# A fused attention, expert routing and two-layer kernel: the second products one block later, the high halves first, and the splitting work at other places

## The chip, the cores and the metric

The kernel is one program on one core of a Trainium2 chip. Five engines work side by side: PE (TensorE, matmuls), DVE (VectorE), ACT (ScalarE), POOL (GpSimd) and SP (SyncE, which here only issues transfers). They wait for each other through semaphores. The metric is the device time of one execution in microseconds (us), the median over the runs; a lower number is better.

## What is computed

```python
# attention with decay, over B=4 batches, H=8 heads, S=768 steps, D=48
for t in range(S):
    cur = einsum('bhd,bhe->bhde', u[None] * kt, vt)
    y[:, :, t] = einsum('bhd,bhde->bhe', rt, state + cur)
    state = w[None, :, :, None] * state + einsum('bhd,bhe->bhde', kt, vt)
x = y.transpose(0, 2, 1, 3).reshape(3072, 384)
# expert layer: 8 experts of exactly 384 tokens, given out by descending logit
logits = x @ w_gate
for idx in argsort(-logits.flatten()):
    tok, e = idx // 8, idx % 8
    if assigned[tok] >= 0 or counts[e] >= 384: continue
    assigned[tok] = e; counts[e] += 1
for e in range(8):
    out[assigned == e] = relu(x[assigned == e] @ w1[e]) @ w2[e]      # 384 -> 1024 -> 384
# common layer
h = relu(out @ w_in)                                                 # 384 -> 2048
out = (h * h) @ w_out                                                # 2048 -> 384
```

## The kernel before

**Attention** goes over 24 units (6 chunks of 128 steps, 4 batches each). For each unit the tensor engine makes the scores, the part from the state and the part inside the chunk; DVE adds them to a row tile `yrow` (`rows`). One unit later `turn` transposes this tile into PSUM bank 6 (`tr_ps`), ACT copies it to `yT` (`turned_y`), `gate` multiplies it with `w_gate` into the end of the same bank (`lg_ps`), and ACT copies the eight logits (`gated`). Since one bank serves all units, `turn` waits until the logits of the unit before have been copied out (`logit_ready`).

**Routing.** Experts are not filled token by token. For the expert that fills up next a threshold on the keys (the logit's bits) is searched in six steps: DVE compares all keys with a ramp of thresholds (`keys`, then `compare`, written to `hot`), the tensor engine counts (`count`), DVE tests the counts (`fullness`), and the tensor engine adds up the result (`add_full`), which the next compare needs. Then `ranks`, `slots`, `slot_hot` and `slot_ids` turn the winners into 384 row numbers (`perm`), and POOL gathers the rows with an indirect DMA (`gather`). The first search stands alone, between attention and the experts. The other six are done during the work of the expert before: five of them in a loop, the last expert needs no search at all.

**Expert stages.** There are eight, which I number 0 to 7. In each, blocks g = 0 to 7 are the expert's own layer and g = 8 to 23 the common layer. `hidden(g)` makes 128 rows of the hidden layer, `contract(g)` multiplies them by the second matrix and adds to three accumulator banks. Every float32 value is split into a high part (what the fast format holds) and a low part (the rest), and each product is made of three matmuls: high times high, high times low, low times high (`three`). One `hidden` or `contract` is thus nine matmuls of 384 columns. ACT makes the high part `h_hi` (`high`), DVE the low part `h_lo` (`low`); for g of 8 and above DVE makes the square `sq` and POOL the low part. Block 24 of a stage is block 0 of the next one.

**What sets the order.** It is written out by hand in one loop over g for each engine, and each engine does its instructions strictly in that order. In the search stages the tensor engine does `count` number g-2 behind block g, for g = 2 to 7, and `add_full` number g-3 inside `hidden(g)`. DVE's loop begins at g = 1 with `low`, `need`, `keys` and the first `compare`.

**Splitting the weights.** Each expert's weights are six tiles of 128 x 1024 in three buffers: SP loads them, ACT makes `w_hi` (`split_high`), DVE `w_lo` (`split_low`). Tiles 0 to 2 are the first matrix (W1_TILES = 3). The common second matrix is split once, in stage 0: `out_low` makes one of twelve halves of 128 x 512 (`m_lo`), and the table `OUT_LOW_AT` says behind which g each stands.

`fill` is a run of matmuls whose result nobody reads; it stands where the tensor engine would idle.

## Time and profile before

| | |
|---|---|
| median of 3 runs | 811.03 us (810.62 to 811.88) |
| the profiled execution: its own time, and its span | 812.36 us, 810.6 us |
| busy in the span: PE, DVE, ACT, POOL | 777.7, 500.7, 321.5, 292.9 us |
| instructions | 19168 |
| mean granted clock of the tensor engine | 0.978 of full |
| tensor engine's part of the chain that ended last | 79% (DVE 10%, "issue" 4%, POOL 3%) |

The span is the time from the first to the last instruction; what the profiled execution's time has beyond it (1.76 us) lies around it. The chain that ended last is the work, followed back from the last instruction, in which each piece released the next. The granted clock is what the chip's throttle gave the tensor engine, 1.00 being the upper of its two levels (2.4 GHz) and 0.50 the lower (1.2 GHz).

### The profile page before, as it was taken

The numbers are of one execution on the slowest core, as the hardware profiler recorded it, in microseconds if no ns is written. First come the engines' busy times: TensorE is split into PE (matmuls) and PEld (weight loads), VectorE is DVE, ScalarE is ACT, GpSimd is POOL, SyncE is SP. The second block draws the span as 40 slices with busy tenths as digits, with TensorE's granted clock in tenths as the row PEclk, the third lists the DMA queues.
The fourth block names the chain that finished last, engine by engine and source line by source line (L and its number), as shares of the span: only waits on it lengthen the run. The fifth ranks groups of instructions, "written<-read, shape, count | busy, mean of one in ns | idle before, by whom it ended". The sixth has DMA issues, their size and how long they took to land.

```text
span 810.6 us, 19168 instructions
## 1 busy us (share of the span) xinstructions
PE 777.7 (96%) x6971; PEld 743.8 (92%) x6971; DVE 500.7 (62%) x1195; ACT 321.5 (40%) x718; POOL 292.9 (36%) x295
## 2 busy tenths in 40 slices
PE   8999994799999999999999999999999999999996
PEld 6999993589899999999999999999999999999995
DVE  7988886788846783678367837783777336721210
ACT  4556654313532353235323532363236324531332
POOL 7766640102631163116311631263126312621333
PEclk9999996699999999999999999999999999999998
DMA  8878744502300140013001300130013002300000
GB/s 227 263 233 239 236 126 177 183 3 79 108 1 30 40 145 0 29 49 136 0 29 51 133 0 29 55 129 0 29 56 128 0 30 79 108 1 30 0 1 30
DMA packets 22196, 65.27 MB, mean 81 GB/s; under 512 B 3664, under 2 KB 6736, under 8 KB 22160
## 3 DMA queue, kind: packets, MB, share of 16 engines
q1 hardware_dynamic: 19088, 55.34, 21.4%
q0 software_dynamic: 3072, 9.44, 3.3%
q8 instruction: 24, 0.39, 0.2%
q14 instruction: 12, 0.10, 0.0%
HBM read 55.33 MB, written 9.44 MB: 80 GB/s over the span
## 4 chain that ended last, share of the span: by engine, by line
PE 79%; DVE 10%; issue 4%; POOL 3%; ACT 1%; DMA 1%; POOLq 0%; SPq 0%; DVEq 0%; ACTq 0%
PE bank L1362 14%; PE bank L1366 14%; PE bank L1363 14%; PE bank L1420 7%; PE bank L1421 7%; PE bank L1422 7%; PE bank L1166 3%; PE bank L1204 3%; PE bank L1179 3%; DVE hot L863 2%; DVE hot L977 1%; PE bank L1233 1%; PE bank L1220 1%; PE bank L1241 1%; POOL xg L476 1%
## 5 line engine op out<-in xcount | busy, mean ns | idle before, releaser
L503 POOL TENSOR_TENSOR h_lo<-sq,h_hi 128x384 fp32r<-128x384 f32 x128 | 155.4, 1217 | 377.3 <-DVE sq L1076 377.2
L1076 DVE SCALAR_TENSOR_TENSOR sq<-bank,relu 128x384 f32<-128x384 f32 x128 | 71.0, 555 | 152.1 <-ACT relu L627 150.1
L627 ACT ACTIVATE relu<-bank 128x384 f32<-128x384 f32 x128 | 62.9, 492 | 196.1 <-PE bank L1366 182.5
L1420 PE MATMUL bank<-m_hi,h_hi 128*128 128x384 f32 x384 | 132.7, 346 | 2.2 <-POOL h_lo L503 2.0
L1362 PE MATMUL bank<-x_hi,m_hi 128*128 128x384 f32 x384 | 129.8, 338 | 0.6
L1421 PE MATMUL bank<-m_lo,h_hi 128*128 128x384 f32 x384 | 130.2, 339 | 0.0
L1366 PE MATMUL bank<-x_hi,m_lo 128*128 128x384 f32 x384 | 130.0, 339 | 0.0
L1422 PE MATMUL bank<-m_hi,h_lo 128*128 128x384 f32 x384 | 129.8, 338 | 0.0
L1363 PE MATMUL bank<-x_lo,m_hi 128*128 128x384 f32 x384 | 128.9, 336 | 0.0
L621 ACT ACTIVATE h_hi<-bank 128x384 fp32r<-128x384 f32 x64 | 31.5, 492 | 175.3 <-PE bank L1366 175.3
L1068 DVE SCALAR_TENSOR_TENSOR h_lo<-bank,h_hi 128x384 fp32r<-128x384 f32 x64 | 35.4, 554 | 73.2 <-ACT h_hi L621 73.2
L1420 PEld LDWEIGHTS bank<-m_hi,h_hi 128*128 128x128 f32 x384 | 72.3, 188 | 4.5 <-POOL h_lo L503 4.5
L1362 PEld LDWEIGHTS bank<-x_hi,m_hi 128*128 128x128 f32 x384 | 72.3, 188 | 2.0 <-DVE x_lo L1096 0.9
L1421 PEld LDWEIGHTS bank<-m_lo,h_hi 128*128 128x128 f32 x384 | 72.5, 189 | 0.0
L1422 PEld LDWEIGHTS bank<-m_hi,h_lo 128*128 128x128 f32 x384 | 72.4, 189 | 0.0
L1366 PEld LDWEIGHTS bank<-x_hi,m_lo 128*128 128x128 f32 x384 | 72.3, 188 | 0.0
L1363 PEld LDWEIGHTS bank<-x_lo,m_hi 128*128 128x128 f32 x384 | 72.3, 188 | 0.0
L629 ACT ACTIVATE h_hi<-relu 128x384 fp32r<-128x384 f32 x128 | 67.2, 525 | 4.0
L1362 PE MATMUL bank<-x_hi,w_hi 128*128 128x384 f32 x192 | 67.3, 351 | 0.5 <-DVE x_lo L1030 0.5
L1366 PE MATMUL bank<-x_hi,w_lo 128*128 128x384 f32 x192 | 67.2, 350 | 0.0
L1362 PE MATMUL bank<-h_hi,w_hi 128*128 128x384 f32 x192 | 64.5, 336 | 1.4 <-DVE h_lo L1068 1.4
L294 DVE TENSOR_TENSOR w_lo<-w_raw,w_hi 128x1024 fp32r<-128x1024 f32 x48 | 63.9, 1334 | 2.1 <-ACT w_hi L597 2.1
(191 smaller groups left out, 1445.3 us busy)
## 6 DMA issues: line engine op xcount, KB each, us to landing
w_raw<-we_in SPq DMA_DIRECT2D x48, 512.0 KB, 5.5
nn<-nn_in SPq DMA_DIRECT2D x24, 384.0 KB, 4.0
tt<-tt_in SPq DMA_DIRECT2D x44, 192.0 KB, 4.3
m_raw<-m_in SPq DMA_DIRECT2D x12, 512.0 KB, 6.1
x_rows<-yrow SPq DMA_DIRECT2D x24, 192.0 KB, 2.2
tt<-tt_in SPq DMA_DIRECT2D x4, 256.0 KB, 5.9
xg<-x_rows,perm_next POOLq DMA_INDIRECT x24, 5.1
out<-xg,perm_now POOLq DMA_INDIRECT x24, 2.6
```

Of the source, the lines that this page charges most:

```text
L294: eng.tensor_tensor(w_lo[:, cols], w_raw[j % W_SLOTS][:, :], w_hi[:, cols].bitcast(f32), ALU.subtract).then_inc(w_lo_ready, 1)
L503: pool.tensor_tensor(h_lo[g % 3][:, :], sq[g % 2][:, :], h_hi[g % 3][:, :].bitcast(f32), ALU.subtract).then_inc(lo2_ready, 1)
L627: act.activation(relu[:, :], h_ps[g % 3][:, 0:CAP], ACT.Relu).then_inc(relu_ready, 1)
L629: act.activation(h_hi[g % 3][:, :], relu[:, :], ACT.Square).then_inc(h_hi_ready, 1)
L1068: dve.scalar_tensor_tensor(out=h_lo[g % 3][:, :], in0=h_ps[g % 3][:, 0:CAP], scalar=0.0, in1=h_hi[g % 3][:, :].bitcast(f32), op0=ALU.max, ...
L1076: dve.scalar_tensor_tensor(out=sq[g % 2][:, :], in0=h_ps[g % 3][:, 0:CAP], scalar=0.0, in1=relu[:, :], op0=ALU.max, op1=ALU.mult).then_inc ...
L1362: pe.matmul(out, hi_w, hi_x, start=first, stop=False)
L1363: pe.matmul(out, hi_w, lo_x, start=False, stop=False)
L1366: return pe.matmul(out, lo_w, hi_x, start=False, stop=last)
L1420: pe.matmul(acc_ps[t][:, 0:DM], h_hi[r][:, s], m2_hi[:, c:c + DM], start=first, stop=False)
L1421: pe.matmul(acc_ps[t][:, 0:DM], h_hi[r][:, s], m2_lo[:, c:c + DM], start=False, stop=False)
L1422: last = pe.matmul(acc_ps[t][:, 0:DM], h_lo[r][:, s], m2_hi[:, c:c + DM], start=False, stop=end)
```

## The change

Six edits.

1. `turn` and `gate` of attention's last unit write to bank 7 (`u_ps`), so that `turn` no longer waits for the logits of the unit before, but for the last state.
2. The keys of the first 20 units are made ahead of the last `rows`, not behind it.
3. The gathered rows of stage 0 are transposed into the accumulator banks instead of the hidden banks, and `fill` uses bank 2.
4. In the expert's own layer `contract` stands two blocks behind `hidden` instead of one, and the last three stand together behind block 7.
5. `hidden` of g = 0 and g = 8 waits for the high half of its input only; the low half is waited for in front of the last of the three products.
6. In stage 0 the three splits of the second matrix stand behind `high(0, 0)` and `low(0, 0)`, and at g = 2 and 4; the twelve `out_low` are placed anew.

```diff
-OUT_LOW_AT = [2, 3, 4, 5, 8, 10, 13, 15, 16, 17, 18, 19]
+OUT_LOW_AT = [8, 8, 8, 10, 10, 10, 17, 17, 18, 18, 19, 19]
...
+        def turned_in(n):
+            return u_ps if isinstance(n, int) and n == NU - 1 else tr_ps
+        def gated_in(n):
+            return turned_in(n)[:, 504:512]
...
-            return (h_ps[d] if is_first(q) else rt_ps if d == 1 else xt_ps)[:, 0:CAP]
+            return (acc_ps[d] if is_first(q) else rt_ps if d == 1 else xt_ps)[:, 0:CAP]
...
             high(0, 0)
-            for j in range(W1_TILES + 1, WE_TILES):
+            for j in range(W1_TILES, WE_TILES):
                 split_high(0, j)
...
                     if last and b == B - 1:
                         pick(slice(0, EARLY), begin=False)
                         need()
+                        keys(slice(0, EARLY))
                     rows(i, b)
...
-                        if is_first(i) and g == 3:
-                            split_low(dve, 0, W1_TILES + 2)
-                        if is_first(i) and g in OUT_LOW_AT:
-                            out_low(dve, OUT_LOW_AT.index(g)).then_inc(out_lo_ready, 1)
+                        if is_first(i) and g in (2, 4):
+                            split_low(dve, 0, W1_TILES + g // 2)
+                        if is_first(i):
+                            for n in range(2 * OUT_TILES):
+                                if OUT_LOW_AT[n] == g:
+                                    out_low(dve, n).then_inc(out_lo_ready, 1)
...
             low(0, 0)
-            split_low(dve, 0, W1_TILES + 1)
+            split_low(dve, 0, W1_TILES)
...
+                elif turned_in(n) is tr_ps:
+                    pe.wait_ge(logit_ready, n)
                 else:
-                    pe.wait_ge(logit_ready, n)
+                    pe.wait_ge(state_ready, NU)
...
                 pe.matmul(out, hi_w, hi_x, start=first, stop=False)
+                if low_ready:
+                    pe.matmul(out, lo_w, hi_x, start=False, stop=False)
+                    pe.wait_ge(*low_ready)
+                    if between:
+                        between()
+                    return pe.matmul(out, hi_w, lo_x, start=False, stop=last)
...
                         if g == 0:
                             pe.wait_ge(w_lo_ready, WE_TILES * i + d + 1)
-                            pe.wait_ge(x_lo_ready, DC * i + d + 1)
+                            pe.wait_ge(x_hi_ready, DC * i + d + 1)
+                            low_ready = x_lo_ready, DC * i + d + 1
...
                         if g == G1:
-                            pe.wait_ge(x2_lo_ready, DC * i + d + 1)
+                            pe.wait_ge(x2_hi_ready, DC * i + d + 1)
+                            low_ready = x2_lo_ready, DC * i + d + 1
...
-                    if g < G1:
+                    if 1 < g < G1:
+                        contract(i, g - 2)
+                    if g == G1 - 1:
                         contract(i, g - 1)
-                    if g == G1 - 1:
                         contract(i, g)
```

**The tensor engine at the head of an expert stage.** Its rows from the top of the loop to the first half of the first count; a row is `line operation output<-inputs columns`, a `hidden` reads `x_hi,w_hi`, a `contract` reads `h_hi,w_hi`, and "..." stands for the other eight matmuls of each. Before:

```order
L1462 UNCONDITIONAL_BRANCH
L1362 MATMUL bank<-x_hi,w_hi 128x384
...
L1362 MATMUL bank<-h_hi,w_hi 128x384
...
L1362 MATMUL bank<-x_hi,w_hi 128x384
...
L1362 MATMUL bank<-h_hi,w_hi 128x384
...
L1300 MATMUL bank<-need,ones 128x8
L1303 REGISTER_ALU
L1304 MATMUL bank<-openc,hot 128x16 x6
```

And of the changed kernel:

```order
L1483 UNCONDITIONAL_BRANCH
L1373 MATMUL bank<-x_hi,w_hi 128x384
...
L1373 MATMUL bank<-x_hi,w_hi 128x384
...
L1373 MATMUL bank<-h_hi,w_hi 128x384
...
L1311 MATMUL bank<-need,ones 128x8
L1314 REGISTER_ALU
L1315 MATMUL bank<-openc,hot 128x16 x6
```

Between the loop's head and the first count stood four groups of nine matmuls; now three. The missing one, a `contract`, stands behind the last block of the expert's layer.

**DVE in stage 0, blocks 8 to 11.** `sq` is the square of a block, `m_lo` an `out_low`, `cand<-r` the last step of `filled` (g = 9), on which `ranks` waits. Before:

```order
L1076 SCALAR_TENSOR_TENSOR sq<-bank,relu 128x384
L288 TENSOR_TENSOR m_lo<-m_raw,m_hi 128x512
...
L938 TENSOR_REDUCE cand<-r 128x24
L1076 SCALAR_TENSOR_TENSOR sq<-bank,relu 128x384
L288 TENSOR_TENSOR m_lo<-m_raw,m_hi 128x512
L1076 SCALAR_TENSOR_TENSOR sq<-bank,relu 128x384
L943 SCALAR_TENSOR_TENSOR pre<-ones,bank 128x48
```

And of the changed kernel:

```order
L1082 SCALAR_TENSOR_TENSOR sq<-bank,relu 128x384
L296 TENSOR_TENSOR m_lo<-m_raw,m_hi 128x512 x3
...
L946 TENSOR_REDUCE cand<-r 128x24
L1082 SCALAR_TENSOR_TENSOR sq<-bank,relu 128x384
L296 TENSOR_TENSOR m_lo<-m_raw,m_hi 128x512 x3
L1082 SCALAR_TENSOR_TENSOR sq<-bank,relu 128x384
L951 SCALAR_TENSOR_TENSOR pre<-ones,bank 128x48
```

Four more halves stand in front of the routing's `slots` (line 943 before) and `slot_hot`; in exchange there is none any more at blocks 2 to 5, 13, 15 and 16.

## Rows read from the trace of the kernel before

**Rows 1.** Work by stretch of time: busy time (x count) per engine, granted clock.
```profile
core 0: us, PE busy (x) PEld busy (x) DVE busy (x) ACT busy (x) POOL busy (x), PEclk, DMA share, GB/s
158.00:168.10 10.10, 8.50 (x57) 7.94 (x58) 7.07 (x15) 4.33 (x6) 0.00 (x0) 1.00 0.37 141
...
219.30:222.80 3.50, 3.50 (x12) 3.50 (x13) 3.42 (x3) 0.53 (x1) 1.72 (x2) 0.51 0.07 28
231.00:311.70 80.70, 80.59 (x531) 77.86 (x530) 51.02 (x130) 30.33 (x56) 26.93 (x23) 1.00 0.15 54
```
**Rows 2.** Weight loads of the tensor engine in time, stage 1: start, length, ..., [idle before].
```profile
246.76 0.19 PEld L1362 LDWEIGHTS bank<-x_hi,w_hi 128*128 128x128 f32 x1
...
251.45 0.19 PEld L1362 LDWEIGHTS bank<-h_hi,w_hi 128*128 128x128 f32 x1
...
253.18 0.10 PEld L1300 LDWEIGHTS bank<-need,ones 128*128 128x128 bf16 x1 [0.16 <-DVE key_lo L835]
...
253.51 0.19 PEld L1362 LDWEIGHTS bank<-x_hi,w_hi 128*128 128x128 f32 x1
```
**Rows 3.** ACT and DVE in order of time in the same stretch of stage 1.
```profile
248.70 0.49 ACT L621 ACTIVATE h_hi<-bank 128x384 fp32r<-128x384 f32 x1 [1.08 <-PE bank L1366]
...
251.17 1.83 DVE L867 TENSOR_TENSOR hot<-key_hi,ramps 128x768 bf16<-128x768 int32 x2
```
**Rows 4.** Stage 0 in order of time, from the last weight tile to the first count.
```profile
162.66 0.19 PEld L1362 LDWEIGHTS bank<-h_hi,w_hi 128*128 128x128 f32 x1 [1.74 <-issue]
...
162.88 1.06 ACT L597 ACTIVATE w_hi<-w_raw 128x1024 fp32r<-128x1024 f32 x1 [0.85 <-DMA w_raw<-we_in]
...
166.09 1.83 DVE L867 TENSOR_TENSOR hot<-key_hi,ramps 128x768 bf16<-128x768 int32 x2
...
167.97 0.21 PEld L1304 LDWEIGHTS bank<-openc,hot 128*128 128x128 bf16 x6 [0.27 <-DVE hot L867]
...
168.11 0.19 PEld L1362 LDWEIGHTS bank<-x_hi,w_hi 128*128 128x128 f32 x1
```
**Rows 5.** The tensor engine's waits in stage 0 behind the first count, timeline.
```profile
177.69 0.11 PEld L1312 LDWEIGHTS bank<-full,ones_times 128*128 128x128 bf16 x2 [1.06 <-DVE folded L889]
...
181.66 0.10 PEld L1312 LDWEIGHTS bank<-full,ones_times 128*128 128x128 bf16 x1 [0.50 <-DVE folded L889]
```
**Rows 6.** Timeline row of stage 0; then waits of the whole span: us, times, longest.
```profile
219.15 0.19 PEld L1420 LDWEIGHTS bank<-m_hi,h_hi 128*128 128x128 f32 x1 [2.27 <-POOL h_lo L503]
...
PEld bank L1420 <- POOL h_lo L503: 4.5, 7, 2.3
```
**Rows 7.** POOL in order of time, gather and next low part, stages 0 and 1.
```profile
212.09 1.62 POOL L476 DMA_INDIRECT xg<-x_rows,perm_next  x1 [0.99 <-DVE open_t L1008]
...
218.10 2.92 POOL L503 TENSOR_TENSOR h_lo<-sq,h_hi 128x384 fp32r<-128x384 f32 x3
...
295.77 1.59 POOL L476 DMA_INDIRECT xg<-x_rows,perm_next  x1 [1.04 <-DVE open_t L1008]
...
300.19 2.14 POOL L503 TENSOR_TENSOR h_lo<-sq,h_hi 128x384 fp32r<-128x384 f32 x2
```
**Rows 8.** DVE and weight loads in stage 0, blocks 8 to 14; last, the halves grouped.
```profile
192.38 0.68 DVE L288 TENSOR_TENSOR m_lo<-m_raw,m_hi 128x512 fp32r<-128x512 f32 x1
...
193.37 0.56 DVE L1076 SCALAR_TENSOR_TENSOR sq<-bank,relu 128x384 f32<-128x384 f32 x1 [0.32 <-ACT relu L627]
...
196.74 0.35 DVE L938 TENSOR_REDUCE cand<-r 128x24 bf16<-128x192 f32 x1
...
197.35 0.10 PEld L1321 LDWEIGHTS bank<-cand,before 128*128 128x128 bf16 x1 [0.16 <-issue]
...
206.92 0.67 PEld L1328 LDWEIGHTS bank<-ids,hot 128*128 128x128 bf16 x24 [0.16 <-DVE hot L977]
...
L288 DVE TENSOR_TENSOR m_lo<-m_raw,m_hi 128x512 fp32r<-128x512 f32 x12 | 10.2, 851 | 0.0
```
**Rows 9.** The tensor engine's last turn in attention, timeline.
```profile
124.63 0.52 PE L1233 MATMUL bank<-ident,yrow 128*128 128x128 f32 x3 [0.43 <-ACT logits L546]
```
**Rows 10.** Weight load at block 8 of stage 6, where nothing is counted.
```profile
674.23 0.19 PEld L1362 LDWEIGHTS bank<-x_hi,m_hi 128*128 128x128 f32 x1 [0.45 <-DVE x_lo L1096]
```

More of the change, by code:

```diff
@@ L223, in build @@
         sc_ps, y_ps, tr_ps, u_ps = bank[0:2], [banks[:, 2 + 2 * j:4 + 2 * j, :] for j in range(2)], bank[6], bank[7]
-        lg_ps, own_ps = tr_ps[:, 504:512], tr_ps[:, 496:504]
+        own_ps = tr_ps[:, 496:504]
+        def turned_in(n):
+            return u_ps if isinstance(n, int) and n == NU - 1 else tr_ps
+        def gated_in(n):
+            return turned_in(n)[:, 504:512]
         h_ps, acc_ps, rt_ps, xt_ps = bank[0:3], bank[3:6], bank[6], bank[7]
@@ L540, in turned_y @@
                     act.wait_ge(logit_sum, n)
-                act.activation(yT[:, :], tr_ps[:, 0:DM], ACT.Copy).then_inc(yT_ready, 1)
+                act.activation(yT[:, :], turned_in(n)[:, 0:DM], ACT.Copy).then_inc(yT_ready, 1)
             def gated(n):
                 act.wait_ge(logit_sum, n + 1)
-                act.activation(logits[:, bass.ds(n, 1), :].rearrange("p o e -> p (o e)"), lg_ps,
+                act.activation(logits[:, bass.ds(n, 1), :].rearrange("p o e -> p (o e)"), gated_in(n),
                                ACT.Copy).then_inc(logit_ready, 1)
@@ L614, in _ @@
                 x_high(0, d)
-            split_high(0, W1_TILES)
             def high(i, g):
@@ L1030, in x_low @@
                 dve.tensor_tensor(x_lo[:, d, :], turned(q, d), x_hi[:, d, :].bitcast(f32), ALU.subtract).then_inc(x_lo_ready, 1)
-            keys(slice(0, EARLY))
             compare(0, 0, "a")
@@ L1061, in _ @@
                 x_low(0, d)
-            split_low(dve, 0, W1_TILES)
             def low(i, g):
@@ L1228, in turn @@
                     pe.wait_ge(own_ready, 2)
+                elif turned_in(n) is tr_ps:
+                    pe.wait_ge(logit_ready, n)
                 else:
-                    pe.wait_ge(logit_ready, n)
+                    pe.wait_ge(state_ready, NU)
                 for d in range(DC):
-                    last = pe.transpose(tr_ps[:, d * P:(d + 1) * P], yrow[b][:, d * P:(d + 1) * P], ident[:, :])
+                    last = pe.transpose(turned_in(n)[:, d * P:(d + 1) * P], yrow[b][:, d * P:(d + 1) * P], ident[:, :])
                 last.then_inc(yT_sum, 1)
@@ L1240, in gate @@
                     for t in range(0, P, HALF):
-                        last = pe.matmul(lg_ps[t:t + HALF, :], yT[:, d * P + t:d * P + t + HALF], wg[:, d, :],
+                        last = pe.matmul(gated_in(n)[t:t + HALF, :], yT[:, d * P + t:d * P + t + HALF], wg[:, d, :],
                                          start=d == 0, stop=d == DC - 1)
@@ L1349, in _ @@
             slot_ids(0)
-            fill(FILLS[0], 1)
+            fill(FILLS[0], 0)
             for t in range(TT):
@@ L1357, in _, with three @@
                         last.then_inc(x_sum, 1)
-                fill(FILLS[t + 1], 1)
-            def three(out, hi_w, lo_w, hi_x, lo_x, first, last, between=None):
+                fill(FILLS[t + 1], 0)
+            def three(out, hi_w, lo_w, hi_x, lo_x, first, last, between=None, low_ready=None):
                 pe.matmul(out, hi_w, hi_x, start=first, stop=False)
+                if low_ready:
[4 more added lines that the diff above has]
+                    return pe.matmul(out, hi_w, lo_x, start=False, stop=last)
                 pe.matmul(out, hi_w, lo_x, start=False, stop=False)
@@ L1373, in hidden @@
                 for d in range(DC):
+                    low_ready = None
                     if g < G1:
@@ L1384, in hidden @@
                         if g == G1:
-                            pe.wait_ge(x2_lo_ready, DC * i + d + 1)
+                            pe.wait_ge(x2_hi_ready, DC * i + d + 1)
+                            low_ready = x2_lo_ready, DC * i + d + 1
                     last = three(h_ps[h][:, 0:CAP], w1[:, c:c + P], w2[:, c:c + P], a1[:, d, :], a2[:, d, :],
-                                 d == 0, d == DC - 1, between if d == DC - 1 else None)
+                                 d == 0, d == DC - 1, between if d == DC - 1 else None, low_ready)
                 last.then_inc(h_sum, 1)
```

## The prediction

> **What bounds the kernel now.** I read the page first: the tensor engine is busy in 777.7 of 810.6 us, and the chain of waits that ended last runs on it for 79%. So the change can only gain where the tensor engine waits, and every new wait on it costs its full length. Next I went through the tensor engine's weight loads in order of time and looked for steps longer than those inside a dense stretch. In stages 1 to 7 there is next to nothing: from 246.76 to 251.45 three groups of nine matmuls take 4.69 us, 1.56 a group or 0.174 a matmul [rows 2]. The waits are in stage 0 and at a few edges: 1.74 us ahead of its first `contract` [rows 4], 1.06 and 0.50 in its search [rows 5], 2.27 for a low part from POOL [rows 6], behind which the clock is at half for one stretch [rows 1], 0.43 at attention's last `turn` [rows 9], and 0.45 at block 8 of stage 6, and the same in stage 7, where no count fills the gap [rows 10]. That is all the change can win. The thing to look at is what waits for the tensor engine and is only just in time, for there a shifted order makes a new wait. Such a place is the first count of a stage.
>
> **The change part by part.** The sum is made against the profiled execution (812.36 us, span 810.6) and then set on the median of 811.03, which lies 1.3 lower.
>
> *Contract two blocks behind, stages 1 to 5.* The first search step of a stage hangs on `hidden(1)`: ACT makes its high part at 248.70, DVE its low part, then `need`, `keys` and the two halves of the first compare from 251.17, which end at 253.00 [rows 3]. The count is started at 253.18 [rows 2], so it came 0.2 us behind its data. Nothing in this chain moves: `hidden(1)` stands at the head of the stage as before. But there is one group of nine less between it and the count. The tensor engine is at the count at 253.18 - 1.56 = 251.62, and stands until the second half is written. From that moment to the next `hidden` stage 0 shows what it takes: end 167.92, count 167.97, next weights 168.11, 0.19 us [rows 4]. The next `hidden` then starts at 253.19 instead of 253.51, with four groups done instead of five: 1.56 - 0.32 = 1.24 us lost. The group that was left out is done behind block 7, where nothing waited for it. Behind the standing count is the whole remaining stage, each step of which (count, test, sum, compare) keeps its distance, so nothing is given back. Stages 1 to 5 have a search: 5 x 1.24 = **+6.2**. Stages 6 and 7 have none and lose nothing here.
>
> *The same in stage 0.* Here the chain to the first compare hangs on something else: `high` of block 1 stands on ACT behind the last weight tile, which comes by DMA and is split at 162.88; the compare runs from 166.09 to 167.92 [rows 4]. The changed order keeps `high(0,1)` behind that tile. So the wait of 1.74 at the first `contract` goes, but the tensor engine then stands at the count, from about 163.5 on, until the same compare. At the next `hidden` it has done one group less: **+1.6**. All this comes earlier by what attention gives, next item.
>
> *Attention's last turn.* It waited 0.43 us for the logits of the unit before [rows 9]; the state and the rows it now waits for are there. Keys ahead of the last `rows` take DVE's idle time and keep it off this chain. **-0.4**, and everything up to the first compare follows, the DMAs of gather and weights too.
>
> *Clock at the new wait.* From 163.5 to 167.5 the tensor engine has nearly nothing to do, longer than the 2.27 us behind which the clock fell [rows 6]. In that stretch 12 matmuls took 3.5 us [rows 1], at 0.174 each they take 2.1, so one such stretch costs 1.4. The 1.74 us in stage 0 did not do it: the clock is 1.00 from 158.0 to 168.1 [rows 1]. I take one stretch lost: **+1.4**; bounds 0 and 2.8.
>
> *Splits in stage 0's search.* Before there was a half at g = 2, a tile and a half at g = 3, a half at g = 4, and the waits were 1.06 (behind g = 3) and 0.50 (behind g = 4) [rows 5]. Now there is a tile at g = 2, none at 3, a tile at g = 4. A half takes 0.68 [rows 8] and a tile has twice the columns, so I take 0.6 more for it: the wait of 1.06 goes, the 0.50 becomes 1.1, and at g = 2 some 0.3 would appear but for the half clock, which gives DVE time. **-0.5**.
>
> *Twelve halves at new places.* Ahead of `ranks` and `slot_ids` in stage 0 there are now six halves instead of two, 4 x 0.68 = 2.7 us, less the 0.32 that DVE idled at 193.37: 2.4 us late. DVE had 0.26 us to spare at `ranks` (197.09 against 197.35) and the tensor engine already waited for `hot` at `slot_ids` [rows 8]. So the tensor engine waits about 2.2 us more there, in two pieces. In return no half stands beside the gather, which took 6.0 us from 212.09 to 218.10 in stage 0 and 4.4 in stage 1 [rows 7]; the wait for the low part behind it falls from 2.27 to what the other six have, (4.5 - 2.3) / 6 = 0.4 [rows 6]. Together 2.2 + 0.4 - 2.3 = **+0.3**. Bounds: -1 if DVE finds the time elsewhere, +1.3 if each half takes the mean of 0.851 [rows 8] and blocks on POOL. The pieces are shorter than the 2.27, so the half-clock stretch goes: **-1.4**.
>
> That the gather is quicker without halves beside it is what the two stages' rows show, no more. The Trainium skill (SBUF — State Buffer, Who interferes with whom) speaks against it: a DVE `tensor_tensor` with both inputs in SBUF shuts out only those GpSimd instructions that read SBUF, and it infers that writing a gather's descriptors is not among them. By the rule the gather would stay at 6.0 us, and the sum would be 1.6 higher.
>
> *High halves first.* At block 8 of stages 6 and 7 the 0.45 goes, with a little on the two blocks of input behind it 0.5 each: **-1.0**. In stages 1 to 5 the count stands there and hides it: 0. The other banks for stage 0's transposes and fills change no wait: 0. If their cover failed it would be the length of one `x_lo`, about 0.5.
>
> Sum: -0.4 + 1.6 + 1.4 - 0.5 + 0.3 - 1.4 + 6.2 - 1.0 = +6.2. On the profiled execution that is 818.6, on the median **817.2 us**, 0.8% slower.
>
> **The rivals.**
> - *Stage 0 comes out cheaper*: no clock lost at the long wait (-1.4), and half of the halves' delay hidden (-1.1). 814.7 us. The rows show 2.27 us of waiting with a fallen clock behind it and 1.74 without, and this wait is cut in two by the first half of the count. Chance 0.17.
> - *The gather is slow for another reason than DVE* (the rule above): its 6.0 us stay, +1.6, 818.8 us. For it: the first piece of the gather took 1.62 and 1.59 us in the two stages, alike with and without a half near it [rows 7]. Chance 0.13.
> - *The clock also falls at the five new waits*: each has 1.24 us of standing plus a count of tiny matmuls. Against it the 1.74 us in stage 0 that left it at 1.00. Between two and five times 1.4: 820 to 824. Chance 0.06.
> - *Faster: the count is not reached early*, because the compare comes sooner than I think. Then only gains are left: -0.4 - 1.7 - 1.6 - 1.9 - 1.4 - 1.0 = -8.0, 803 us. It needs the second half of the compare by 251.8 instead of 253.0, and every piece of that chain is behind `hidden(1)`, so I see no way. It decides from 0.4 us of wait per stage downwards. Chance 0.07.
> - *No change*: the new wait is about half of what I take (0.5 us in each of six stages), which balances the gains. Chance 0.05.
>
> **How the numbers follow.** The forecast has 0.52, its own range is 815.5 to 818.8 (clock at the long wait, halves). The range that leaves out no more than 0.2 goes from the cheap stage 0 with a margin, 813.8, to the slow gather with one more stretch of clock, 819.8. Slower by over 0.2% (1.6 us, about what a measurement of this kernel can tell from no change) are the first three cases and the forecast: 0.88. Within it 0.05, faster 0.07.
>
> **What would show it.** In the changed kernel's profile, at the first count of stages 1 to 5, a wait of the tensor engine of 1.0 to 1.3 us for `hot<-key_hi,ramps`; in stage 0 no wait at the first `contract` but one of 3 to 4 us, in two pieces, at the first count, and a stretch of half clock behind it; waits of about 0.6 and 1.6 us at `ranks` and `slot_ids` of stage 0, and 0.4 for the low part behind the gather, at full clock. Stages 1 to 5 should take 81.9 us each instead of 80.7 [rows 1], stages 6 and 7 0.5 less. I am wrong if the search stages keep their length; then the chain behind `hidden(1)` was not what the count waited for.

## The result, and the profile after

The changed kernel takes 821.38 us (median of 4 runs, 819.49 to 822.17) against 811.45 for the kernel before, run beside it: a ratio of 1.0111, with a 95% interval of 1.0093 to 1.0129. (Ratios here are taken over all the runs of a pair and not from the two medians, whose quotient would be 1.0122.) It is slower by 1.1%. One execution of a kernel further down, of 951 us at a mean granted clock of 0.745, is left out of its ratio as a slow one. The profiled execution took 821.92 us, its span is 820.2.

The page's row of busy times, then stretches of the span as busy time and granted clock: attention's routing, stage 0's own layer, a stretch in it, stage 0's common layer, a stretch in it, and stage 1.

```profile
PE 781.4 (95%) x6971; PEld 746.7 (91%) x6971; DVE 506.0 (62%) x1195; ACT 321.3 (39%) x718; POOL 293.6 (36%) x295
```
```profile
core 0: us, PE busy (x) PEld busy (x) DVE busy (x) ACT busy (x) POOL busy (x), PEclk, DMA share, GB/s
129.30:153.10 23.80, 12.50 (x185) 9.72 (x186) 16.94 (x61) 9.45 (x9) 2.28 (x3) 0.50 0.44 163
157.15:192.64 35.49, 31.32 (x204) 28.64 (x203) 23.08 (x66) 8.51 (x16) 0.00 (x0) 0.90 0.12 45
166.80:173.60 6.80, 6.11 (x30) 5.71 (x31) 4.70 (x13) 0.49 (x1) 0.00 (x0) 0.50 0.01 2
192.64:248.66 56.02, 53.07 (x323) 51.70 (x320) 43.65 (x76) 23.45 (x42) 23.72 (x19) 0.97 0.19 68
214.60:218.00 3.40, 3.40 (x13) 3.40 (x12) 3.30 (x10) 0.00 (x0) 1.18 (x1) 0.51 0.40 130
248.66:330.45 81.79, 80.79 (x531) 77.98 (x530) 51.16 (x129) 30.21 (x55) 26.93 (x23) 1.00 0.15 53
```

Both kernels go through the same layers, so the span can be cut at the first weight load of each layer (the windows above begin 0.05 us behind it) and compared piece by piece. This table is worked out so, in us, from the two traces; the last piece ends at the last weight load, and 8.6 us follow in either trace:

| piece | before | after | difference |
|---|---|---|---|
| start to stage 0's first `hidden` | 157.83 | 157.10 | -0.73 |
| stage 0, own layer | 31.39 | 35.49 | +4.10 |
| stage 0, common layer | 54.40 | 56.02 | +1.62 |
| stages 1 to 5, each | 80.72 | 81.77 | +1.05, five times +5.24 |
| stages 6 and 7 | 154.84 | 154.13 | -0.71 |

They add up to the difference of the spans, 9.5 us. Stages 1 to 5 first, weight loads in order of time in stage 1, the counterpart of [rows 2].

```profile
248.61 0.19 PEld L1373 LDWEIGHTS bank<-x_hi,w_hi 128*128 128x128 f32 x1
...
256.61 0.10 PEld L1311 LDWEIGHTS bank<-need,ones 128*128 128x128 bf16 x1 [0.16 <-issue]
257.16 0.22 PEld L1315 LDWEIGHTS bank<-openc,hot 128*128 128x128 bf16 x6 [0.45 <-DVE hot L875]
258.03 0.22 PEld L1315 LDWEIGHTS bank<-openc,hot 128*128 128x128 bf16 x6 [0.65 <-DVE hot L875]
258.18 0.19 PEld L1373 LDWEIGHTS bank<-x_hi,w_hi 128*128 128x128 f32 x1
```
The count is reached 8.00 us behind the stage's start (256.61 - 248.61) and now stands twice, for each half of the compare. This is the foreseen wait, at the foreseen place.

Stage 0 the same way: the tensor engine's weight loads, then ACT, then DVE, around the first count, beside [rows 4].

```profile
162.00 0.19 PEld L1373 LDWEIGHTS bank<-h_hi,w_hi 128*128 128x128 f32 x1
...
165.44 0.10 PEld L1311 LDWEIGHTS bank<-need,ones 128*128 128x128 bf16 x1 [1.90 <-DVE need L826]
...
166.95 0.24 PEld L1315 LDWEIGHTS bank<-openc,hot 128*128 128x128 bf16 x6 [1.42 <-DVE hot L875]
167.82 0.23 PEld L1315 LDWEIGHTS bank<-openc,hot 128*128 128x128 bf16 x6 [0.63 <-DVE hot L875]
...
162.76 1.06 ACT L605 ACTIVATE w_hi<-w_raw 128x1024 fp32r<-128x1024 f32 x1 [0.91 <-DMA w_raw<-we_in]
163.72 0.85 ACT L628 ACTIVATE h_hi<-bank 128x384 fp32r<-128x384 f32 x2
...
164.22 0.56 DVE L1074 SCALAR_TENSOR_TENSOR h_lo<-bank,h_hi 128x384 fp32r<-128x384 f32 x1 [2.35 <-ACT h_hi L628]
...
165.94 1.83 DVE L875 TENSOR_TENSOR hot<-key_hi,ramps 128x768 bf16<-128x768 int32 x2
```
The first `contract` no longer waits (162.00). But `high` of block 1 stands on ACT behind the last weight tile, DVE idles 2.35 us for it with `need`, `keys` and the compare still ahead of it in its list, and the tensor engine stands 1.90 + 1.42 + 0.63 = 3.95 us. Behind that the clock is at its lower level (0.50) for 6.8 us, twice as long as the one stretch that I had counted.

In stage 0's common layer: waits of weight loads, the three halves at each of two blocks on DVE, and POOL beside them.

```profile
197.97 0.19 PEld L1440 LDWEIGHTS bank<-m_hi,h_hi 128*128 128x128 f32 x1 [0.54 <-issue]
202.14 0.10 PEld L1332 LDWEIGHTS bank<-cand,before 128*128 128x128 bf16 x1 [1.09 <-DVE cand L946]
213.61 0.27 PEld L1339 LDWEIGHTS bank<-ids,hot 128*128 128x128 bf16 x8 [1.33 <-DVE hot L985]
228.81 0.19 PEld L1440 LDWEIGHTS bank<-m_hi,h_hi 128*128 128x128 f32 x1 [0.96 <-POOL h_lo L511]
...
195.75 2.71 DVE L296 TENSOR_TENSOR m_lo<-m_raw,m_hi 128x512 fp32r<-128x512 f32 x3
202.47 2.71 DVE L296 TENSOR_TENSOR m_lo<-m_raw,m_hi 128x512 fp32r<-128x512 f32 x3
...
196.02 1.30 POOL L511 TENSOR_TENSOR h_lo<-sq,h_hi 128x384 fp32r<-128x384 f32 x1 [39.25 <-DVE sq L1082]
202.71 1.32 POOL L511 TENSOR_TENSOR h_lo<-sq,h_hi 128x384 fp32r<-128x384 f32 x1 [2.61 <-DVE sq L1082]
```
Together 3.92 us of wait, where there was one of 2.27 [rows 6]. Three halves took 2.71 us, not 3 x 0.68 = 2.04. The three are merged in the rows above; one by one, the first and the third took 0.68 and the second, which began while a low part of POOL was running, 1.50:

```profile
196.35 1.50 DVE L296 TENSOR_TENSOR m_lo<-m_raw,m_hi 128x512 fp32r<-128x512 f32 x1
```
The first half of each three (195.75) began 0.27 us before POOL's low part (196.02) and wasn't longer for it. And behind the wait of 1.33 at `slot_ids` the clock falls again (214.6 to 218.0, 0.51), so the half-clock stretch that was to vanish has only moved.

### The profile page after: what moved, and what is told of

Same layout as the page of the kernel before. It is cut to its first block, busy times and chain, and to the rows that moved or that the text cites. A ratio compares the mean times of both kernels' runs of the same rounds, so it can differ in the third digit from the quotient of the medians.

```text
span 820.2 us, 19168 instructions
## 1 busy us (share of the span) xinstructions
PE 781.4 (95%) x6971; PEld 746.7 (91%) x6971; DVE 506.0 (62%) x1195; ACT 321.3 (39%) x718; POOL 293.6 (36%) x295
## 4 chain that ended last, share of the span: by engine, by line
PE 67%; DVE 17%; issue 8%; POOL 4%; ACT 2%; DMA 1%; DVEq 0%; POOLq 0%; SPq 0%; ACTq 0%
PE bank L1373 12%; PE bank L1383 11%; PE bank L1380 11%; PE bank L1440 5%; PE bank L1441 5%; PE bank L1442 5%; DVE hot L985 3%; PE bank L1174 3%; PE bank L1212 3%; DVE sq L1082 2%; PE bank L1187 2%; DVE w_lo L302 2%; POOL xg L484 1%; PE bank L1244 1%; PE bank L1228 1%
## 5 line engine op out<-in xcount | busy, mean ns | idle before, releaser
L1383 PE MATMUL bank<-x_hi,m_lo 128*128 128x384 f32 x360 | 121.6, 338 | 0.0
L1380 PE MATMUL bank<-x_lo,m_hi 128*128 128x384 f32 x360 | 121.1, 336 | 0.0
L1383 PEld LDWEIGHTS bank<-x_hi,m_lo 128*128 128x128 f32 x360 | 67.9, 189 | 0.0
L1380 PEld LDWEIGHTS bank<-x_lo,m_hi 128*128 128x128 f32 x360 | 67.9, 189 | 0.0
L302 DVE TENSOR_TENSOR w_lo<-w_raw,w_hi 128x1024 fp32r<-128x1024 f32 x48 | 66.0, 1378 | 0.4 <-ACT w_hi L605 0.4
L1383 PE MATMUL bank<-h_hi,w_lo 128*128 128x384 f32 x192 | 64.8, 338 | 0.0
```

The source lines that it names most:

```text
L302: eng.tensor_tensor(w_lo[:, cols], w_raw[j % W_SLOTS][:, :], w_hi[:, cols].bitcast(f32), ALU.subtract).then_inc(w_lo_ready, 1)
L1380: pe.matmul(out, hi_w, lo_x, start=False, stop=False)
L1383: return pe.matmul(out, lo_w, hi_x, start=False, stop=last)
```

## Experiments

Each kernel was measured beside the kernel before on the same chip, whose median lay between 811.7 and 812.2 us. "The changed kernel" below is the one after. All lengths of layers are cut as in the table above, from the one trace of each kernel. The quoted texts were written before each run; a label in them is given in the heading of its kernel.

**1. Contractions one block behind again.** In the changed kernel:
```
-                    if 1 < g < G1:
-                        contract(i, g - 2)
+                    if g < G1:
+                        contract(i, g - 1)
                     if g == G1 - 1:
-                        contract(i, g - 1)
                         contract(i, g)
```


> The changed kernel with contract one block behind again, all else as changed. Theory (the first count of a stage is reached one group of nine matmuls too early and stands for the compare): stages 1 to 5 go from 81.8 us back to 80.7 (-5.3), stage 0 gets its group back ahead of the count (-1.6) and loses one of the two half-clock stretches behind the long wait (-1.3): about 813.3 us, 812.3 to 814.5. Rival (the time is lost to the added waits of the high-halves-first hidden, nine matmuls with a wait inside): stages 1 to 5 stay at 81.8 and the time stays above 819.

815.00 us, ratio 1.0046 (1.0030 to 1.0063). Stages 1 to 5 are 80.62 us long, so the loss there is the order's, all of it. But stage 0's own layer stays at 35.36, against my expectation, and so the time lies above its range. Its weight loads show another wait, and the windows the clock behind it:
```profile
161.21 0.19 PEld L1373 LDWEIGHTS bank<-h_hi,w_hi 128*128 128x128 f32 x1 [1.59 <-issue]
...
171.26 0.19 PEld L1373 LDWEIGHTS bank<-h_hi,w_hi 128*128 128x128 f32 x1 [2.35 <-DVE w_lo L302]
```
```profile
171.30:174.30 3.00, 3.00 (x16) 2.70 (x16) 0.38 (x1) 0.00 (x0) 0.00 (x0) 0.55 0.00 0
```
With the old order the moved weight split (tile 4 at g = 2) is what `contract(2)` waits for, the first block that reads this tile. With these places of the splits the old order has that wait of 2.35 us, and the new order has not.

**2. The order alone, on the kernel before** (the reverse of that diff).

> The kernel before with one edit, contract two blocks behind. Theory: a standing of the tensor engine of about 1 us at the first count of stages 1 to 5 and 1.06 us more per stage (+5.3), in stage 0 one group (+1.6) and half-clock stretches behind a wait of about 4 us (+1.4 to +2.8), less its wait in the search (-0.5 to -1): 818.8 to 820.5 us. Rival (the order alone is neutral, other edits make the loss): 811 to 813.

820.23 us, ratio 1.0110 (1.0091 to 1.0129): as slow as the whole change. Stages 1 to 5 are 81.75 us long, stage 0's own layer 34.45 (+3.06), its common layer 54.43 (+0.03). The order alone costs as much as the whole change. In stage 0 its +3.06 is what the prediction had for it (+1.6 and +1.4), with one half-clock stretch of 3.4 us behind the first count. The rest of the change is not free for all that: kernel 1 has it without the order and is slower by 0.46%. So the costs of the parts don't add up.

**3. The old table of the halves, in the changed kernel.**
```
-OUT_LOW_AT = [8, 8, 8, 10, 10, 10, 17, 17, 18, 18, 19, 19]
+OUT_LOW_AT = [2, 3, 4, 5, 8, 10, 13, 15, 16, 17, 18, 19]
```


> The changed kernel with the old table of the twelve halves, all else as changed. Theory (six halves ahead of ranks and slot_ids in stage 0 delay DVE by 3.5 us there): the waits of 1.1 at ranks and 1.3 at slot_ids fall to 0.2 or less, that at the gather rises to about 2.3, and the search in stage 0 gets about 1 us of waits back; the sum is -1 to -2, 819.4 to 820.4 us. Rival (the halves cost what they cost wherever they stand): 821.4, within 0.5.

819.16 us, ratio 1.0098 (1.0081 to 1.0115), 2.2 us less than the changed kernel by the medians, with intervals of the ratios that overlap; the lengths of the layers show where it comes from. The common layer of stage 0 falls from 56.02 to 52.88, the own layer, in which four halves stand again, grows from 35.49 to 36.33. So the new table costs, where I had it at +0.3 with a clock stretch of 1.4 won back. Of the 3.14 us of the common layer some 1.1 are the clock, which is 1.00 throughout this one.

**4. The stage's first needs ahead of block 1's split on DVE**, in the changed kernel:
```
                 for g in range(1, G if last else G + 1):
+                    if not last and g == 1:
+                        need()
+                        if search:
+                            keys()
                     low(i, g)
-                    if not last and g == 1:
-                        need()
-                        if search:
-                            keys()
```


> The changed kernel with need and keys ahead of low(1) on DVE instead of behind it, so that the chain from hidden(1) to the first compare is 1.35 us shorter while the order of the products stays two behind. Theory: the standing at the first count of stages 1 to 5 goes to about 0, they take 80.7 or a little less (-5.3), and stage 0 loses about 1.3 us of its wait and may lose one half-clock stretch (-1.3 to -2.7): 813.4 to 815 us. Rival (added waits inside hidden, or the order as such): no change, above 820.

816.67 us, ratio 1.0057 (1.0037 to 1.0077). Stages 1 to 5 are 81.35 us, only 0.42 less; the tensor engine still waits for the compare, which still follows `low`. Stage 0's own layer is 33.27, with one half-clock stretch instead of two. More was won than the rival allowed and less than the theory said.

**5. The first compare too** (`compare_first`). As 4, with `compare(0, 0)` behind `keys()`.

> The changed kernel with the need, the keys and the first comparison all ahead of the split of hidden block 1 on VectorE (with need and keys alone moved it took 816.7 us, and its stages 1 to 5 were 81.35 us long, 0.62 more than before's 80.73). Theory (what is left of the loss in stages 1 to 5 is the wait of the first counts for the comparison on VectorE): those stages are 80.6 to 80.9 us, some 3.0 us less in all, and stage 0 wins 0.5 to 1.2: 812.5 (812.0 to 813.5); if the half-clock stretch behind stage 0's first count goes too, 809.5 to 811. Rival (the comparison ahead only puts the wait off to contraction 1, which then waits for its split): 816 to 818.

810.73 us, ratio 0.9985 (0.9972 to 0.9998). (In the profiled execution of this kernel attention alone took 7 us longer than in any other; its expert stages are read here, its total is not.) Weight loads at the first count of stage 1:
```profile
257.15 0.10 PEld L1311 LDWEIGHTS bank<-need,ones 128*128 128x128 bf16 x1 [0.16 <-issue]
257.17 0.52 PEld L1315 LDWEIGHTS bank<-openc,hot 128*128 128x128 bf16 x12
257.61 0.19 PEld L1373 LDWEIGHTS bank<-x_hi,w_hi 128*128 128x128 f32 x1
```
No wait is left at this count. But the next step of the search now waits for DVE, which makes two `low` between the compare and its test:

```profile
259.43 0.10 PEld L1323 LDWEIGHTS bank<-full,ones_times 128*128 128x128 bf16 x1 [0.46 <-DVE folded L897]
```
Stages 1 to 5 are 80.91 us on average, 0.86 less than in the changed kernel and still 0.3 more than in kernel 1, which has the old order (80.62). Stage 0's own layer is 30.37 at full clock, 5.12 less than in the changed kernel, 2.2 of which are clock (kernel 13). In the total, moving a few DVE instructions ahead of one gives back the change's loss. `contract(1)` does not wait for its later split, as the rival had it.

**6. The old places of the weight splits**, in the changed kernel (on ACT and DVE tile 3 ahead of block 0, on DVE tile 4 behind it and tile 5 at g = 3).

> The changed kernel with stage 0's own last three weight tiles split where before had them (on ScalarE one ahead of hidden block 0, on VectorE one ahead of it, one behind it, one behind block 3). Theory (these splits matter little; the order of the contractions makes stage 0's long wait): -0.3 to -1.0, 820.4 to 821.2. Rival (the moved splits are what makes hidden block 0 and the first count late, and so the second half-clock stretch): 816.5 to 818.5, and no second half-clock stretch at 170 us.

818.64 us, ratio 1.0079 (1.0049 to 1.0110). Stage 0's own layer is 34.03, 1.46 less: the new places cost there, they do not win the 0.5 that I had put. The waits at the first count stay nearly as long (1.53 + 1.42 + 0.65), but only one half-clock stretch follows them, from 168.0 to 171.4 us: the second one is gone, as the rival had it, though the time is 0.1 us beyond its range. At 2.17 us for two (kernel 13), some 1.1 of the 1.46 are that stretch, an estimate; what is left for the splits themselves is small. The total can't be told from the changed kernel's, the intervals overlap.

**7. The high halves first, alone**, on the kernel before (with the other banks for stage 0's turned rows and fills).

> The kernel before with the high-half products first, the turned rows in the accumulators' banks and the filling products in bank 0; order, splits and table as before. Theory (0.36 us won in each of stages 6 and 7, up to 0.1 in each of 1 to 5, nothing in stage 0): 811.0 (810.4 to 811.4) against a before of 811.8, a ratio of 0.999. Rival (the shorter hidden blocks at a stage's start bring a later wait, so nothing is won): 811.6 to 812.2.

811.86 us, ratio 0.9989 (0.9978 to 1.0001). In the trace stages 6 and 7 are 0.35 us shorter each and 1 to 5 0.13; the sum, 1.3 us, is about what the total can resolve.

**8. High halves and attention part**, on the kernel before.

> The kernel before with the high-half products first and with the attention part of the change (last unit turned and gated in another bank, its keys sooner); order, splits and table as before. Theory (the bank wins 0.4 us more, the early keys take the first comparison's wait down): 810.6 (810.0 to 811.2). Rival (the 0.45 us won at the bank is lost again, as the changed kernel's attention took as long as before's): the same as with the high halves alone, within 0.2 us.

811.20 us, ratio 0.9987 (0.9973 to 1.0001). Not to be told from 7 in the total. Stage 0's first `hidden` starts at 157.4 to 157.8 us in the three traces without the attention part and at 156.0 to 157.5 in the twelve with it (the one of 5 left out). So a few tenths are likely, no more can be said. In this trace, though nothing of the order is changed, the stretch from 162.3 to 168.0 us has a clock of 0.70 behind a wait of 2.35 us at the first `contract`.

**9. The halves spread** (`compare_table`), on kernel 5: `OUT_LOW_AT = [3, 5, 6, 6, 8, 13, 16, 17, 18, 18, 19, 20]`.

> compare_first (810.7 us) with the twelve halves of the output layer spread, at blocks 3, 5, 6, 6, 8, 13, 16, 17, 18, 18, 19, 20, so that no three stand at one block and the one at block 18 keeps its neighbours. Theory (of the halves' three at a block come the 0.5 us wait at block 8, the 1.1 us one at the ranks and the 1.3 us one at slot_ids): 808.7 (808.0 to 809.8), stage 0's common layer 52.5 to 53.5 us long instead of 54.9. Rival (the waits only move to where the halves now stand): 810.3 to 811.3.

807.12 us, ratio 0.9946 (0.9934 to 0.9959). Stage 0's common layer is 51.53 us. Both lie below the ranges of the theory, and the kernel beats both the changed one and the one before.

**10. Kernel 5 with before's table** (`compare_old`).

> compare_first (810.7 us) with before's table of the twelve halves. In the changed kernel the old table made stage 0's own layer 0.8 us longer and its common layer 3.1 us shorter, of which some 1.4 us was the clock kept at contraction 14's wait. Theory: 809.6 (808.8 to 811.0), 2.3 us of wait for h_lo behind the gather as before. Rival (with the first count no longer late, the halves at blocks 2 to 5 make it so again): 811.5 to 813.

809.85 us, ratio 0.9982 (0.9971 to 0.9992). Common layer 52.86, as in 3, own layer 31.66.

**11. Kernel 10 with before's weight splits too.**

> compare_first (810.7 us) with before's table and before's places of stage 0's own last three weight splits: what is left of the change are the order of the contractions, the high halves first and the attention part. Theory (with VectorE's comparison early, contractions two blocks behind cost nothing): 809.0 to 810.5, the same as before's order with high halves and attention part (811.2) or up to 2 us better. Rival (the order costs by itself, whatever VectorE does first): 812.5 to 815.

811.88 us, ratio 1.0013 (1.0002 to 1.0025), between theory and rival. Own layer 32.22, common layer 54.44. So with the compare early the new places of the splits win some 0.6 us in the own layer, and the common layer has its half-clock stretch back: 0.79 from 216 to 224 us.

**12. Kernel 10, `high` of block 1 ahead of the last own weight tile on ACT** (stage 0 is written out ahead of ACT's loop for it).

> compare_old with ScalarE taking hidden block 1's high half ahead of stage 0's last own weight tile, whose load it waits for. Theory (that high half is what makes hidden block 1's split, and with it the fold of the first count, late): 0.5 to 1.0 us below compare_old, 808.0 to 810.0. Rival (VectorE's own list decides, ScalarE waits there for nothing): within 0.3 us of compare_old.

810.45 us, ratio 1.0006 (0.9980 to 1.0032). The own layer is 31.59 instead of 31.66: nothing. With the compare early, that high part is waited for by nobody.

**13. The wait filled**, in the changed kernel, stage 0 alone: 15 products of 256 columns into a free bank ahead of the wait for `need`, 9 behind the product of `need`. For this the tensor engine's stage 0 is taken out of its loop and written out, a second edit.
```
+                    if isinstance(q, int) and q == 1:
+                        for _ in range(15):
+                            pe.matmul(h_ps[0][:, 0:256], ones[:, :], ...
                     pe.wait_ge(route_done, q * RN + DONE["need"])
                     pe.matmul(need_ps, ones[:, :], need8[:, :], start=True, stop=True)
+                    if isinstance(q, int) and q == 1:
+                        for _ in range(9):
+                            pe.matmul(h_ps[0][:, 0:256], ones[:, :], ...
...
             hidden(0, 0)
-            with pe.Fori(0, E - 2) as i:
+            expert(0, False, True)
+            with pe.Fori(1, E - 2) as i:
                 expert(i, False, True)
```


> The changed kernel with stage 0's first count filled as the attention's end is: 15 products of 256 columns whose result nobody reads ahead of the wait for the need, and 9 behind the product of the need (some 0.11 us each, in the waits of 1.9 and 1.3 us). Theory (the half-clock stretch from 166.8 to 173.6 us is a loss of its own beside the waits): the waits stay, the stretch goes, and 5.6 us of products at half rate become shorter by up to 2.8: 819.0 (818.2 to 820.4) against 821.4. Rival (what the clock loses there VectorE would have cost anyway, as each later count waits for it): 820.8 to 822.

818.32 us, ratio 1.0078 (1.0062 to 1.0094). Weight loads, then the same window as in the changed kernel:
```profile
163.61 1.53 PEld L1312 LDWEIGHTS bank<-ones 128*128 128x128 bf16 x15 [0.16 <-issue]
165.34 0.10 PEld L1314 LDWEIGHTS bank<-need,ones 128*128 128x128 bf16 x1 [0.20 <-DVE need L826]
165.36 0.89 PEld L1317 LDWEIGHTS bank<-ones 128*128 128x128 bf16 x9
166.85 0.21 PEld L1321 LDWEIGHTS bank<-openc,hot 128*128 128x128 bf16 x6 [0.61 <-DVE hot L875]
```
```profile
166.80:173.60 6.80, 6.01 (x49) 5.28 (x50) 5.55 (x19) 0.49 (x1) 0.00 (x0) 1.00 0.00 0
```
`need` and compare come as late as ever, but the clock is 1.00 where it was 0.50, with 49 matmuls in the window for 30. The own layer falls from 35.49 to 33.32: I read the 2.17 us as what the clock cost. Writing stage 0 out was not run by itself; kernel 14 has it too, and its stage 0 is no shorter than that of kernel 9 (own layer 30.70 for 30.47, common layer 51.61 for 51.53). The common layer is 1.10 shorter too (54.92), with the same waits (1.3 at `slot_ids`) and no fallen clock behind them; nothing was changed there but this writing out.

**14. Each order where it pays.** Two blocks behind, and the compare early on DVE, in stage 0 alone; before's order in the other stages; the spread table of 9.

> The contractions two blocks behind, and VectorE's need, keys and first comparison ahead of block 1's split, in stage 0 alone; stages 1 and later in before's order on both engines; high halves first, attention part and the spread table as in compare_table (807.1 us). Theory (compare_table's stages 1 to 5 are 80.86 us long against 80.60 with before's order and the high halves): 805.8 (805.3 to 806.4). Rival (the two orders need stage 0 written out by itself on TensorE, which costs what the stages win): 806.8 to 808.

806.23 us, ratio 0.9934 (0.9916 to 0.9951). The two layers of stage 0 and stage 1:
```profile
156.39:187.09 30.70, 29.00 (x204) 26.21 (x203) 25.13 (x70) 8.63 (x16) 0.00 (x0) 1.00 0.14 53
187.09:238.70 51.61, 50.98 (x323) 50.05 (x320) 36.98 (x72) 23.57 (x42) 23.74 (x19) 1.00 0.22 74
238.70:319.30 80.60, 80.53 (x530) 77.79 (x529) 51.02 (x129) 30.23 (x55) 26.93 (x23) 1.00 0.16 55
```
The fastest kernel here, 15 us below the changed one and 0.7% below the kernel before. In stage 1 the tensor engine is busy in 80.53 of 80.60 us. By its trace each of stages 1 to 5 wins 0.24 us over 9 (80.62 for 80.86); the medians differ by 0.9 with overlapping intervals, so against 9 it is likely, not shown by the time.

## Why the prediction was right in sign and too small

The direction and its mechanism held: the contraction that was taken out ahead of the first count was what covered the compare on DVE, and five stages pay for it. The size was outside the range: 821.4 us against 817.2 and a range that ended at 819.8, or +9.5 us between the two traces against +6.2. The step that failed is the cost of the twelve halves at their new places, with the clock that was to come back there (-1.1 put, +1.6 found); next to it stand the clock and the splits in stage 0's own layer (+2.5 put, +4.1 found). By the prediction's own steps:

- **Contract two blocks behind, stages 1 to 5**: +6.2 put, +5.2 found in the changed kernel and +5.15 by the order alone (kernel 2). At the count itself the loss is the 1.24 put: from the stage's start to the `hidden` behind the first half of the count it is 9.57 us (258.18 - 248.61) with four groups done, 9.89 before with five, so 1.56 - 0.32 = 1.24. But some 0.2 us comes back in the rest of the own layer, where I had said that nothing would. Kernel 5 shows that the wait was for DVE's list: with the compare moved ahead, the five stages return to 80.91. The 0.3 above kernel 1's 80.62 goes with the wait that moved to the next step.
- **The same in stage 0, clock at the new wait, splits in stage 0's search**: +1.6 + 1.4 - 0.5 = +2.5 put, +4.10 found. Two terms failed. The clock was put at one stretch; it was two in a row (6.8 us), and kernel 13 puts it at 2.17 us, inside the bounds of 0 and 2.8 but not the value taken. Without the clock the layer is 1.93 us longer than before (33.32 against 31.39), so beside the group's 1.6 the splits come to about +0.3, an estimate, where -0.5 was put. The waits in the search changed as foreseen: the 1.06 went and the other became 1.04. But the second half-clock stretch goes with the splits' places: kernel 2, which has the order and the old places, and kernel 6 have one stretch there, the changed kernel and kernel 3 two. Why is not shown.
- **Twelve halves at new places**: this is the step that failed most. +0.3 and -1.4 for the clock, so -1.1, were put, +1.62 found. I costed four more halves ahead of `ranks` and `slot_ids` at 0.68 each, 2.7 us; six took 2 x 2.71 = 5.42 for 2 x 0.68 before, which is 4.06 more. The tensor engine waited 0.54 + 1.09 + 1.33 ahead of the gather, 2.96, where 2.2 was put, and 0.96 behind it where 0.4 was. The step also said that the pieces are shorter than 2.27 and so the stretch goes. It came back behind 1.33. The prediction's 0.68 was a row that also stood beside POOL's low part, but began before it. The mean of 0.851, which it took for its upper bound only, holds a half of 1.49 at 206.66 us and one of 1.90 at 219.68 that began while a low part was running. With the clock kept and the new table the common layer is 54.9 (kernels 5, 6 and 13), with the old table 52.9 (3 and 10). So the table costs 2.0 us, where +0.3 was put, and the clock lost behind the waits is 1.1 where 1.5 was lost before, so -0.4 where -1.4 was put.
- **Gather without halves beside it**: the gather is quicker, by 1.2 us where 1.6 was put. POOL, gather and next low part, of the changed kernel, then of kernel 3, which has the halves back beside it:

```profile
218.31 1.62 POOL L484 DMA_INDIRECT xg<-x_rows,perm_next  x1 [0.99 <-DVE open_t L1016]
220.23 1.60 POOL L484 DMA_INDIRECT xg<-x_rows,perm_next  x1 [0.31 <-DVE sq L1082]
222.14 0.96 POOL L484 DMA_INDIRECT xg<-x_rows,perm_next  x1 [0.30 <-issue]
223.12 2.00 POOL L511 TENSOR_TENSOR h_lo<-sq,h_hi 128x384 fp32r<-128x384 f32 x2
```
```profile
215.18 1.61 POOL L484 DMA_INDIRECT xg<-x_rows,perm_next  x1 [1.00 <-DVE open_t L1016]
...
221.19 2.93 POOL L511 TENSOR_TENSOR h_lo<-sq,h_hi 128x384 fp32r<-128x384 f32 x3
```
  The gather takes 4.81 us from its start to the next low part, against 6.01 in kernel 3 and in the kernel before [rows 7]. Only the table differs between the two. That it is the halves themselves is not shown: the third piece took 1.90 us in kernel 3 (219.27 to 221.17) with no half beside it, and in kernel 9 the gather took 4.61 with a half (212.40) beside it. The table also moves DVE's splits of the next weights, which stand beside the gather in all of them. The Trainium skill (SBUF — State Buffer, Who interferes with whom) infers that a DVE `tensor_tensor` does not hinder the writing of a gather's descriptors; by that the gather would have stayed at 6.0 us. The measurement speaks against it here, since the gather's time changed with the places of such DVE instructions alone.
- **Attention's last turn**: -0.4 put, -0.73 in the one pair of traces, and between nothing and 1.9 over all of them; the total can't tell it from nothing (kernels 7 and 8).
- **High halves first**: -1.0 put, -0.71 found in stages 6 and 7. In before's order it also wins 0.13 us in each of stages 1 to 5 (kernel 7), where 0 was put. With the contractions two blocks behind nothing of that is seen: these stages are 81.77 us with the high halves first and 81.75 without (kernel 2).

Of the rivals, stage 0 came out dearer and not cheaper; the slow gather fell; the clock did not fall at the five waits of stages 1 to 5 (1.00 from 248.66 to 657.40 us), but in stage 0's common layer, which no rival had.

I read the two misses as one mistake. I took each edit of stage 0 by itself and at one clock, while DVE's work there (the search, then `ranks` to `slot_ids`) had next to no slack: of 4.06 us of added halves 2.96 came out as waits of the tensor engine, with the clock's share on top.

## What to carry to other kernels

Before taking a group of matmuls out from ahead of a point where the tensor engine needs a result, look for how little that result is early: here 0.2 us was all. Moving the producer's instructions ahead of a split that nobody waited for yet gave back 0.86 us of each of the five stages; leaving the order alone there gave back 1.15 and is what the fastest kernel does, with the new order only in stage 0. Price work that is moved onto a busy engine by rows that began beside the same neighbours: here a half took 0.68 us or 1.50, by whether it began before POOL's low part or during it. Where a long wait can't be taken away, some idle products ahead of it can be cheaper than the clock that it costs (2.17 us in kernel 13).

## What the runs showed of the hardware

The granted clock is not told by a wait alone. The same wait of 2.27 us for POOL's low part, at the same place of the program, was followed by half clock in the kernel before [rows 1, 6] (0.51), in kernel 2 (0.50 from 223.2 to 226.6 us) and in kernels 7, 8 and 11, but by 1.00 in kernels 3, 10 and 12. The wait of 1.3 us at `slot_ids` was followed by 0.51 in the changed kernel, and by 1.00 in kernels 1, 4, 5, 6 and 13 with the same waits. What decides between them stays open. It also differs between executions of one kernel: kernel 4 took 814.64 us at a mean granted clock of 0.984 and 816.5 to 817.0 at 0.977 to 0.981, and the kernel before, measured beside the others, had 0.981 in 50 of 76 executions, while its profiled one had 0.978. So the half-clock stretches of a trace, the one that the prediction wanted to win back too, need not be those of most executions. In the traces one stretch is worth 1.1 to 1.5 us (52.88 against 54.40 us of common layer in kernel 3 and before, the tensor engine busy in 50.92 of it against 52.45), so in a sum a wait like these two should carry both values.

```profile
192.35:245.23 52.88, 50.92 (x323) 50.06 (x320) 37.45 (x72) 23.67 (x42) 24.48 (x19) 1.00 0.21 72
```
```profile
189.27:243.67 54.40, 52.45 (x318) 51.59 (x319) 37.34 (x72) 23.47 (x42) 24.47 (x19) 0.97 0.20 70
```
The rows are the common layer of stage 0 in kernel 3 and in the kernel before: the same work, 1.5 us more of busy time (five tiny matmuls of a count fall on the other side of the cut, 318 for 323).
